# Loading an expert's first rows during the attention loop, and dropping the constant products before the experts

## The chip, the cores and the metric

The kernel runs on one core of a Trainium2 chip. A core has five engines with an instruction stream each: TensorE (PE in the profile, its weight loads PEld), VectorE (DVE), ScalarE (ACT), GpSimd (POOL) and SyncE (SP), which here only issues transfers. They share an on-chip memory (SBUF) and the matmul accumulators (PSUM), and meet at semaphores. 16 DMA engines move data to and from main memory. The metric is the device time of one execution in microseconds (us). The kernel before takes 883.68 us, the median of three runs (883.65 to 884.09).

## The reference

```python
scores = matmul(z, z.T) / S                  # per batch: 3072 x 64 times 64 x 3072
x = u * matmul(maximum(scores, 0)**2, v)     # 8 batches x 3072 rows x 256 columns

logits = x @ w_gate                          # 8 experts
e_i, gate_i = argmax(logits), softmax(logits)[argmax]
# rows in order: row i takes the next place of expert e_i while counts[e_i] < 768,
# rows that find their expert full give an output of zero
h = maximum(disp[e] @ w1[e], 0)              # 768 x 256 times 256 x 1024
y = h @ w2[e]                                # 768 x 1024 times 1024 x 256
out[i] = gate_i * y[e_i, place_i]            # for the rows that were kept
```

An expert takes 768 rows at most. Once all eight are full, every later row has an output of zero, and attention for it needn't be computed.

## The kernel before

The 24576 rows of x are computed in groups of 384 rows (GROUP, three tiles of 128), eight groups to a batch. Matmuls take fp32 numbers as pairs of fp16 numbers (high and low parts). The program has two parts.

**The attention loop.** Each engine runs the same loop over groups n (`attention_loop`, line 213). Group 0 is peeled off. In pass n, TensorE computes the attention of group n in 12 steps c (scores for three steps ahead at lines 612 and 613, weighted sums at 647 to 651), ScalarE and VectorE turn scores into weights (434, 438, 916, 922), and beside it the rows finished in the pass before are routed: VectorE splits them (1014), SP transposes them by DMA (`xT`, line 263, three transfers), TensorE takes the logits in step 3 (line 688, waiting for `loaded_xT`), VectorE finds each row's place (1050 to 1088) and GpSimd scatters the rows with their gate weight and row number into `disp` in main memory (line 352). VectorE also writes a flag into `ends`: zero once all experts are full. Every engine reads it (`load_end`, line 222), and the loop is left after step 5 of the pass that finds them full. With these inputs that is pass 18 of 64.

SP's pass, in its order: wait for the split rows, three `xT` transposes, load of `ubuf` (264), in each eighth pass the next batch's z and v (277, 282) and a wait for them, in passes 1 to 8 zeros over an eighth of the output (298, 3 MB each), in passes 3 and 5 the weights of experts 0 and 1 (252, 254), a wait for `ubuf`, `load_end`, and in the last pass a wait until all scatters have landed. All of SP's transfers go through one DMA queue (q1 in the profile).

**The experts.** `disp` holds 16 halves of 384 rows, two for each expert. After the loop SP loads the first four (`load_rows`, 313): 384 rows transposed into `xt[:, k]` (line 315), then their gate weights and row numbers into `tail` (317). `xt` and `tail` lie in `vS`, which attention reads until its end, so that SP waits for `pe_over` first. TensorE waits until all engines have left attention (`attention_over` is 3), then does `hidden` (763) and `output` (786 to 790) in turns: the first needs `loaded_x0`. ScalarE and VectorE split the hidden values, GpSimd scatters the results to `out`.

**Constant products.** `turn_over(times)` (line 616) multiplies an identity by ones into a spare part of PSUM, and nobody reads the result. There are 138 at the program's start, 44 after the last attention matmul (`close`) and 36 after the wait for the other engines.

Of the kernel before, what the change touches and what calls it, by code (L numbers as in the profile page):

```python
# [12 lines left out]
F32 = mybir.dt.float32  # L13
# [9 lines left out]
P = 128  # L23
# [20 lines left out]
def relu2_attention_moe(nc, u, v, z, w_gate, w1, w2, out, disp, capacity):  # L44
# [12 lines left out]
    with ExitStack() as ctx:  # L57
# [12 lines left out]
        vS = sb("vS", [P, 2 * CHUNK, 2 * D], F16)  # L70
        rawv = sb("rawv", [P, CHUNK, D], F32)
        rawz = sb("rawz", [P, S // 2], F32)
        zsq = sb("zsq", [P, S // 2], BF16)
        attn = sb("attn", [P, BUFS, 2, GROUP], F32)
        attn_hi = sb("attn_hi", [P, BUFS, 2, GROUP], F16)
# [43 lines left out]
        row = sb("row", [P, 1], F32)  # L119
        least = sb("least", [P, 1], F32)  # L120
        ends = sb("ends", [1, NG], I32)

        identf = sb("identf", [P, P], F32)
        identh = sb("identh", [P, P], F16)
        before = sb("before", [P, P], F16)
        ones = sb("ones", [P, P], F16)
# [16 lines left out]
        fac = sb("fac", [P, 4, TILES], F32)  # L143

        over_s = vS[:, :, :].rearrange("p c d -> p (c d)")
        xt = over_s[:, 0:4 * 2 * DC * GROUP].rearrange("p (b m n) -> p b m n", b=4, m=2 * DC)
        tail = over_s.bitcast(F32)[:, 4 * DC * GROUP:4 * DC * GROUP + 4 * TILES * 2].rearrange(
            "p (b t d) -> p b t d", b=4, t=TILES)
        blank = over_s.bitcast(F32)[:, BLANK_AT * D:BLANK_AT * D + FILL_ROWS * XW].rearrange("p (r d) -> p r d", r=FILL_ROWS)
# [28 lines left out]
        def y_part(t):  # L178
# [11 lines left out]
            wpart_ready wmax_ready wallmax_ready wscale_ready whi_ready wlo_ready w_step  # L190
            loaded_x0 loaded_x1 loaded_x2 loaded_x3 loaded_t0 loaded_t1 loaded_t2 loaded_t3
            h_ready hh_done hl_done y_summed y_ready y_scattered0 y_scattered1 y_scattered2
            y_scattered3 fac_ready h_first hh_first"""
        s = {n: sem(n) for n in names.split()}
        consts = s["consts"]

# [42 lines left out]
        @block.sync  # L239
        def _(sp):  # L240
            for h in range(2):
                sp.dma_start(rawz[:, h * SLICE * P:(h + 1) * SLICE * P], z[0, :, h * SLICE * P:(h + 1) * SLICE * P]
                             ).then_inc(s[f"loaded_z0{h}"], 16)
            for q, name in enumerate("abcde"):
                sp.dma_start(rawv[:, V0_PIECES[q]:V0_PIECES[q + 1], :], v[0, :, V0_PIECES[q]:V0_PIECES[q + 1], :]
                             ).then_inc(s["loaded_v0" + name], 16)
            sp.wait_ge(s["loaded_v0e"], 16)
            sp.dma_start(wg[:, :, :], w_gate).then_inc(s["loaded_wg"], 16)

            def load_expert(e, par):  # L250
                e = e & (E - 1)
                sp.dma_start(wraw1[par][:, :, :], w1[bass.ds(e, 1), :, :].rearrange("a (c p) f -> p (a c) f", p=P)
                             ).then_inc(s[f"loaded_w{par}"], 16)
                sp.dma_start(wraw2[:, par, :, :], w2[bass.ds(e, 1), :, :, :].rearrange("a p c d -> p (a c) d")
                             ).then_inc(s[f"loaded_w{par}"], 16)

            def body(n, end):
                g = n & 7
                if not isinstance(n, int):

                    for t in range(TILES):
                        wait_apart(sp, s["rows_lo"], n * TILES - TILES + 1 + t)
                        sp.dma_start_transpose(xT[:, t, :, :], halves[:, t, 0:2 * D]).then_inc(s["loaded_xT"], 16)
                sp.dma_start(ubuf[:, :, :], u[bass.ds(n & (NG - 1), 1), :, :, :].rearrange("a p t d -> p (a t) d")
                             ).then_inc(s["loaded_u"], 16)
                def load_batch():

                    nxt = ((n + 8) & 56) // 8
                    for key in ("khi_ready", "klo_ready"):  # L270
                        if isinstance(n, int):
                            sp.wait_ge(s[key], 8)
                        else:
                            wait_apart(sp, s[key], (n & 120) + 8)
                    if not isinstance(n, int):
                        wait_apart(sp, s["split_ready"], (n & 120) + 8)
                    sp.dma_start(rawz[:, :], z[bass.ds(nxt, 1), :, :].rearrange("a p n -> p (a n)")
                                 ).then_inc(s["loaded_zv"], 16)
                    for q in range(SLICES):
                        if isinstance(n, int):  # L280
                            sp.wait_ge(s["split_ready"], 2 * q + 2)
                        sp.dma_start(rawv[:, q * SLICE:(q + 1) * SLICE, :],
                                     v[bass.ds(nxt, 1), :, q * SLICE:(q + 1) * SLICE, :].rearrange("a p c d -> p (a c) d")
                                     ).then_inc(s["loaded_zv"], 16)
                    wait_apart(sp, s["loaded_zv"], (n & 120) * 10 + 80)
                if isinstance(n, int):
                    rows = E * capacity // P
                    dv = disp.rearrange("(p r) d -> p r d", p=P)
                    sp.wait_ge(s["blank_ready"], 1)
                    for q in range(rows // FILL_ROWS):  # L290
                        sp.dma_start(dv[:, q * FILL_ROWS:(q + 1) * FILL_ROWS, :], blank
                                     ).then_inc(s["disp_filled"], 16)
                only_if(sp, g == 0, load_batch)
                if not isinstance(n, int):
                    def zero_out():

                        rows = B * S // 8
                        sp.dma_start(out[bass.ds(((n - 1) & 7) * rows, rows), :].rearrange("(p r) d -> p r d", p=P),
                                     empty[:, 0:D].unsqueeze(1).to_broadcast([P, rows // P, D])
                                     ).then_inc(s["out_zeroed"], 16)  # L300
                    only_if(sp, n <= 8, zero_out)
                if not isinstance(n, int):
                    only_if(sp, n == 3, lambda: load_expert(0, 0))
                    only_if(sp, n == 5, lambda: load_expert(1, 1))
                wait_apart(sp, s["loaded_u"], n * 16 + 16)
                load_end(sp, n, end)
                if not isinstance(n, int):
                    only_if(sp, sp.snap(end) < 1, lambda: wait_apart(sp, s["scattered"], n * 48))
                    only_if(sp, n == NG, lambda: sp.wait_ge(s["scattered"], NG * 48))
            attention_loop(sp, body)  # L310
            sp.wait_ge(s["pe_over"], 1)

            def load_rows(at, k):

                sp.dma_start_transpose(xt[:, k, :, :], disp_halves[bass.ds(at, GROUP), 0:2 * D]
                                       ).then_inc(s[f"loaded_x{k}"], 16)
                sp.dma_start(tail[:, k, :, :], disp[bass.ds(at, GROUP), D:D + 2].rearrange("(t p) d -> p t d", p=P)
                             ).then_inc(s[f"loaded_t{k}"], 16)

            for k in range(4):  # L320
                load_rows(k * GROUP, k)
            with sp.Fori(0, E // 2 - 1) as i:
                for k in range(4):
                    j = i * 4 + k
                    if k % 2 == 0:

                        wait_apart(sp, s["wlo_ready"], (i * 2 + k // 2 + 1) * 4)
                        load_expert(i * 2 + k // 2 + 2, k // 2)

                    wait_apart(sp, s[f"y_scattered{k}"], i * 48 + 48)  # L330
                    load_rows((j + 4) * GROUP, k)
# [249 lines left out]
        def _(pe):  # L581
# [54 lines left out]
            def body(n, end, par):  # L636
# [76 lines left out]
                def close():  # L713

                    for t in range(TILES):
                        nc.tensor.matmul(o_part(t), attn_hi[:, END_AT % BUFS, 0, t * P:(t + 1) * P],
                                         vS[:, par * CHUNK + END_AT, 0:D], start=False, stop=True,
                                         skip_group_check=True)
                    turn_over(44)
                    for register in (stop0, stop1, stop):  # L720
                        pe.reg_mov(register, 0)
                both_parts(pe, n, end, part, close)
# [17 lines left out]
            pe.drain().then_inc(s["pe_over"], 1)  # L740
            pe.sem_inc(s["attention_over"], 1)
            pe.wait_ge(s["attention_over"], 3)
            turn_over(36)

            pe.sem_inc(s["y_summed"], TILES)

            def hidden(i, k, p):
# [12 lines left out]
                for fi in range(2):  # L760
                    f = 2 * p + fi
                    for at, (w, x, m) in enumerate(terms):
                        ins = nc.tensor.matmul(Sp[:, 2 * (p % 2) + fi, 0:GROUP], w[par][:, m, f * P:(f + 1) * P],  # L763
                                               xt[:, k, x + m, :], start=(at == 0), stop=(at == len(terms) - 1))
                    if isinstance(q, int) and q == 0 and fi == 0:
                        ins.then_inc(s["h_first"], 1)
                ins.then_inc(s["h_ready"], 1)
# [45 lines left out]
        def _(dve):  # L813
# [17 lines left out]
                    for r in range(0, P, 32):  # L831
                        dve.tensor_scalar(row[r:r + 32, :], quad[r:r + 32, 0:1], float(r), None, ALU.add)
            dve.tensor_scalar(identh[:, :], col, row[:, 0:1], None, ALU.is_equal)
            dve.tensor_scalar(identf[:, :], col, row[:, 0:1], None, ALU.is_equal)
            dve.tensor_scalar(before[:, :], col, row[:, 0:1], None, ALU.is_gt)
            for t in range(TILES):
                dve.tensor_scalar(xrow[:, t, D + 1:D + 2].bitcast(I32), row[:, 0:1], float(t * P - GROUP), None, ALU.add)
# [131 lines left out]
            def body(n, end):  # L969
# [21 lines left out]
                def part(start, stop):  # L991
                    for c in range(start, stop):
# [18 lines left out]
                        if not peeled and c == ROWS_LO_AT:  # L1011
                            for t in range(TILES):
# [2 lines left out]
                                                               scalar=rscale[:, t:t + 1], in1=halves[:, t, 0:D],  # L1015
                                                               op0=ALU.mult, op1=ALU.subtract)
                                ins.then_inc(s["rows_lo"], 1)
                        if peeled and c == GATE_AT[0]:
                            dve.wait_ge(s["loaded_wg"], 16)
                            dve.tensor_reduce(gmx[:, :], wg[:, :, :], AX.XY, ALU.max, apply_absolute_value=True  # L1020
# [240 lines left out]
RSCALE_AT = 0  # L1261
ROWS_HI_AT = 1
ROWS_LO_AT = 0
LOGITS_AT = (3, 2)
COUNTS_AT = (4, 1)
EXP_AT = 4
# [59 lines left out]
```

## Time and profile before

| what | value |
| --- | --- |
| median of three runs | 883.68 us |
| profiled execution, its time | 883.7 us |
| its span, first to last instruction | 881.9 us |
| TensorE busy | 863.2 us, 98% of the span |
| VectorE busy | 631.5 us, 72% |
| ScalarE busy | 573.5 us, 65% |
| attention loop ends (last weighted sum) | about 616 us |
| experts begin (first hidden matmul) | 624.8 us |

The 1.8 us between the profiled execution's time and its span lie outside the span. "Busy" of TensorE holds the constant products too. A share of busy time says little here: what counts is who is waited for at a place.

### The profile page before, as it was taken

Reading aid. Unit: us, or ns where it says so; the run is one execution under the profiler, and the core shown is the slowest. Engines: PE = TensorE matmul, PEld = TensorE weight load, DVE = VectorE, ACT = ScalarE, POOL = GpSimd, SP = SyncE. Lnnn points to the kernel's source line nnn. Section 1 sums busy time; section 2 is a strip of 40 time slices with the busy share of each in tenths; the row PEclk is TensorE's granted clock in tenths of the full one; section 3 lists DMA queues with packets and bytes.
Section 4 is the critical chain, followed back from the end, with each engine's and each line's share of the span. In section 5 each row is a group of like instructions: output and inputs, shape, how many; then the busy total and the mean of one; then the engine's idle time right before and its main releaser. Section 6 shows DMA issues by size and latency. Waiting matters only on the chain.

```text
span 881.9 us, 22816 instructions
## 1 busy us (share of the span) xinstructions
PE 863.2 (98%) x7373; PEld 689.7 (78%) x7374; DVE 631.5 (72%) x1346; ACT 573.5 (65%) x874; POOL 122.5 (14%) x121
## 2 busy tenths in 40 slices
PE   6999999999999999999999999999899999999997
PEld 5887887888888887888888888888577777777776
DVE  7976777888888888788788887777265665655531
ACT  6968786768768669787777876776154444434422
POOL 0001101101101110110110110110012112121212
PEclk9999999999999999999999999999999999999999
DMA  8833625635642750110121013311714235325100
GB/s 297 335 101 132 196 83 208 196 96 195 196 126 77 258 155 23 42 50 22 36 54 36 18 52 86 138 42 36 171 37 151 56 129 167 101 77 155 54 18 36
DMA packets 101014, 97.85 MB, mean 111 GB/s; under 512 B 63885, under 2 KB 88538, under 8 KB 99968
## 3 DMA queue, kind: packets, MB, share of 16 engines
q1 hardware_dynamic: 96096, 84.92, 31.4%
q0 software_dynamic: 4896, 12.64, 4.0%
q8 instruction: 13, 0.21, 0.1%
q14 instruction: 9, 0.07, 0.0%
HBM read 40.03 MB, written 44.93 MB: 96 GB/s over the span
## 4 chain that ended last, share of the span: by engine, by line
PE 91%; DVE 3%; issue 3%; ACT 1%; DMA 1%; POOL 0%; ACTq 0%; DVEq 0%; POOLq 0%; SPq 0%
PE O L647 15%; PE O L651 15%; PE O L649 15%; PE Sc L763 14%; PE Sc L612 8%; PE Sc L613 8%; PE O L786 3%; PE O L788 3%; PE O L790 3%; PE M L788 2%; PE M L786 2%; PE M L790 2%; PE M L688 1%; DVE attn_hi L916 0%; ACT Sc L434 0%
## 5 line engine op out<-in xcount | busy, mean ns | idle before, releaser
L647 PE MATMUL O<-vS,attn_hi 128*128 128x256 f16 x1332 | 363.0, 273 | 1.8 <-DVE vS L905 1.6
L651 PE MATMUL O<-vS,attn_lo 128*128 128x256 f16 x1332 | 363.1, 273 | 0.0
L649 PE MATMUL O<-vS,attn_hi 128*128 128x256 f16 x1332 | 363.0, 273 | 0.0
L434 ACT ACTIVATE Sc<-Sc 128x768 f32<-128x768 f32 x224 | 177.9, 794 | 93.1 <-PE Sc L613 72.0
L922 DVE TENSOR_TENSOR attn_lo<-attn,attn_hi 128x768 f16<-128x768 f32 x224 | 214.7, 958 | 7.7
L438 ACT ACTIVATE attn<-Sc 128x768 f32<-128x768 f32 x224 | 181.6, 811 | 7.1
L647 PEld LDWEIGHTS O<-vS,attn_hi 128*128 128x128 f16 x1332 | 130.3, 98 | 29.1 <-issue 1.8
L649 PEld LDWEIGHTS O<-vS,attn_hi 128*128 128x128 f16 x1332 | 130.3, 98 | 26.5
L612 PE MATMUL Sc<-zP 128*128 (+1 forms) x450 | 146.5, 326 | 3.4 <-issue 2.1
L916 DVE CAST attn_hi<-attn 128x768 f16<-128x768 f32 x224 | 125.0, 558 | 32.5 <-ACT attn L438 28.3
L613 PE MATMUL Sc<-zQ,zP 128*128 (+1 forms) x450 | 146.4, 326 | 0.0
L651 PEld LDWEIGHTS O<-vS,attn_lo 128*128 128x128 f16 x1332 | 130.3, 98 | 15.2
L1216 DVE SCALAR_TENSOR_TENSOR rawv<-Sc,rawv 128x768 f16<-128x768 f32 x63 | 60.2, 956 | 114.1 <-ACT rawv L543 72.0
L352 POOL DMA_INDIRECT disp<-xrow,slot x54 | 69.4, 1285 | 475.9 <-DVE slot L1087 442.2
L543 ACT ACTIVATE rawv<-Sc 128x768 f16<-128x768 f32 x63 | 51.0, 810 | 101.1 <-PE Sc L763 98.4
L763 PE MATMUL Sc<-vS,w1h 128*128 128x384 f16 x512 | 105.4, 329 | 2.3 <-DMA vS<-disp 2.3
L763 PEld LDWEIGHTS Sc<-vS,w1h 128*128 128x128 f16 x512 | 50.4, 99 | 31.2 <-DMA vS<-disp 2.5
L786 PE MATMUL O<-w2s,rawv 128*128 128x256 f16 x256 | 69.8, 273 | 0.0
L790 PE MATMUL O<-w2s,rawv 128*128 128x256 f16 x256 | 69.8, 273 | 0.0
L788 PE MATMUL O<-w2s,rawv 128*128 128x256 f16 x256 | 69.8, 273 | 0.0
L387 POOL DMA_INDIRECT out<-attn,vS x48 | 46.9, 977 | 123.1 <-ACT attn L555 109.3
L612 PEld LDWEIGHTS Sc<-zP 128*128 128x128 f16 (+1 forms) x450 | 43.9, 98 | 24.0 <-issue 6.0
(151 smaller groups left out, 890.4 us busy)
## 6 DMA issues: line engine op xcount, KB each, us to landing
out<-empty SPq DMA_DIRECT2D x8, 3072.0 KB, 12.0
wraw<-in_moe_w SPq DMA_DIRECT2D x16, 1024.0 KB
rawv<-in_v SPq DMA_DIRECT2D x14, 768.0 KB, 7.5
ubuf<-in_u SPq DMA_DIRECT2D x19, 384.0 KB, 3.1
disp<-vS SPq DMA_DIRECT2D x8, 774.0 KB, 9.2
rawz<-in_z SPq DMA_DIRECT2D x3, 768.0 KB
xT<-xrow SPq DMA_TRANSPOSE x54, 2.4
disp<-xrow,slot POOLq DMA_INDIRECT x54
```

The costliest lines, as they stand in the source:

```text
L434: act.activation(pair, pair, ACT.Relu).then_inc(s["relu_done"], 1)
L438: act.activation(attn[:, c % BUFS, :, :], Sp[:, 2 * (c % 2):2 * (c % 2) + 2, 0:GROUP], ACT.Square, scale=ROOT_C).then_inc(s["square_done"], 1)
L612: nc.tensor.matmul(to, keys, zP[:, bass.ds(qb, GROUP)], start=True, stop=False)
L613: ins = nc.tensor.matmul(to, keys, zQ[:, bass.ds(qb, GROUP)], start=False, stop=True)
L647: nc.tensor.matmul(o_part(t), hi, v[:, 0:D], start=c == 0 and j == 0 and t % 2 == 0, stop=False, skip_group_check=True)
L649: nc.tensor.matmul(o_part(t), hi, v[:, D:2 * D], start=False, stop=False, skip_group_check=True)
L651: ins = nc.tensor.matmul(o_part(t), lo, v[:, 0:D], start=False, stop=c == PAIRS - 1 and j == 1, skip_group_check=True)
L763: ins = nc.tensor.matmul(Sp[:, 2 * (p % 2) + fi, 0:GROUP], w[par][:, m, f * P:(f + 1) * P], xt[:, k, x + m, :], start=(at == 0), stop=(at ...
L786: nc.tensor.matmul(y_part(t), hi, w2s[:, par, f, 0:D], start=f == 0, stop=False, skip_group_check=True)
L788: nc.tensor.matmul(y_part(t), hi, w2s[:, par, f, D:2 * D], start=False, stop=False, skip_group_check=True)
L916: dve.tensor_copy(attn_hi[:, b, :, :].rearrange("p j n -> p (j n)"), attn[:, b, :, :].rearrange("p j n -> p (j n)")).then_inc(s["hi_done"], 1)
L922: dve.tensor_tensor(attn_lo[:, b, :, :], attn[:, b, :, :], attn_hi[:, b, :, :], ALU.subtract).then_inc(s["lo_done"], 1)
```

## The change

A buffer `x0` of its own takes the rows of expert 0's first half. SP loads it in every pass from 1 on, at the end of the pass's transfers, and waits for the load. Ahead of the load it waits until as many scatters have landed as the register `due` says. VectorE writes that number in step 1 of each pass: 48 for each earlier pass (a pass scatters three tiles, 16 counts each), and 48 more if expert 0 still had under 384 rows when this pass began. The last pass's load is the one that is used. After the loop SP only raises `loaded_x0`, and then loads tail 0 and the rows and tails of halves 1 to 3 as before. The wait for the last scatters stands behind the loop. The 44 and 36 constant products are gone (the 138 at the start stay), and so is `identf`, a second identity that no instruction reads.

```diff
+        x0 = sb("x0", [P, 2 * DC, GROUP], F16)
...
-        identf = sb("identf", [P, P], F32)
...
-        xt = over_s[:, 0:4 * 2 * DC * GROUP].rearrange("p (b m n) -> p b m n", b=4, m=2 * DC)
+        xt = [x0[:, :, :]] + [over_s[:, b * 2 * DC * GROUP:(b + 1) * 2 * DC * GROUP].rearrange("p (m n) -> p m n", m=2 * DC)
+                              for b in range(1, 4)]
...
                 wait_apart(sp, s["loaded_u"], n * 16 + 16)
+                if not isinstance(n, int):
+
+                    wait_apart(sp, s["due_ready"], n * 2)
+                    sp.reg_load(due, dues[0:1, bass.ds((n - 1) & (NG - 1), 1)])
+                    wait_apart(sp, s["scattered"], sp.snap(due))
+                    sp.reg_mov(due, n * 48)
+                    sp.dma_start_transpose(x0[:, :, :], disp_halves[0:GROUP, 0:2 * D]).then_inc(s["loaded_early"], 16)
+                    wait_apart(sp, s["loaded_early"], n * 16)
                 load_end(sp, n, end)
-                if not isinstance(n, int):
-                    only_if(sp, sp.snap(end) < 1, lambda: wait_apart(sp, s["scattered"], n * 48))
-                    only_if(sp, n == NG, lambda: sp.wait_ge(s["scattered"], NG * 48))
...
             attention_loop(sp, body)
+            sp.sem_inc(s["loaded_x0"], 16)
+            wait_apart(sp, s["scattered"], sp.snap(due))
             sp.wait_ge(s["pe_over"], 1)
...
-            for k in range(4):
+            load_tail(0, 0)
+            for k in range(1, 4):
                 load_rows(k * GROUP, k)
...
-                    turn_over(44)
...
-            turn_over(36)
-
             pe.sem_inc(s["y_summed"], TILES)
...
-            dve.tensor_scalar(identf[:, :], col, row[:, 0:1], None, ALU.is_equal)
...
+                        if not peeled and c == DUE_AT:
+
+                            dve.tensor_scalar(lacking[:, :], base[0:1, 0, 0:1], float(GROUP), 48.0, ALU.is_lt, ALU.mult
+                                              ).then_inc(s["due_ready"], 1)
+                            dve.wait_ge(s["due_ready"], n * 2 - 1)
+                            dve.scalar_tensor_tensor(out=dues[0:1, bass.ds((n - 1) & (NG - 1), 1)],
+                                                     in0=xrow[0:1, 0, D + 1:D + 2].bitcast(I32), scalar=48.0 / GROUP,
+                                                     in1=lacking[:, :], op0=ALU.mult, op1=ALU.add
+                                                     ).then_inc(s["due_ready"], 1)
...
+DUE_AT = 1
```

SP's stream from the wait for `ubuf` to the first load behind the loop, before (ISA and the ALU rows are waits and register work, `ends` is the flag):

```order
L201 ISA
L227 REGISTER_ALU x2
L227 ISA
L227 TENSOR_LOAD ends
L210 COMPARE_AND_BRANCH
L201 REGISTER_ALU
L210 UNCONDITIONAL_BRANCH
L210 COMPARE_AND_BRANCH
L210 UNCONDITIONAL_BRANCH
L219 REGISTER_ALU
L219 COMPARE_AND_BRANCH
L315 DMA_TRANSPOSE vS<-disp 128x4x384
```

The same stretch after (the lines of the changed kernel are numbered otherwise, and `x` is `x0`):

```order
L204 ISA
L204 REGISTER_ALU
L312 REGISTER_ALU x2
L312 ISA
L312 TENSOR_LOAD dues
L314 ISA
L315 DMA_TRANSPOSE x<-disp 128x4x384
L230 REGISTER_ALU
L230 TENSOR_LOAD ends
L222 REGISTER_ALU
L222 COMPARE_AND_BRANCH
L327 DMA vS<-disp 128x3x2
```

The row load now stands inside the loop, ahead of the flag's read, and is run in every pass; the first transfer behind the loop is tail 0.

TensorE's stream from the closing attention matmuls to the first hidden ones, before:

```order
L716 MATMUL O<-vS,attn_hi 128x256 x3
L619 MATMUL O<-ones,identh 128x128 x44
L235 UNCONDITIONAL_BRANCH
L737 REGISTER_ALU
L737 COMPARE_AND_BRANCH
L736 UNCONDITIONAL_BRANCH
L739 ISA
L727 COMPARE_AND_BRANCH
L619 MATMUL O<-ones,identh 128x128 x36
L763 MATMUL Sc<-vS,w1h 128x384 x4
L763 MATMUL Sc<-vS,w1l 128x384 x2
```

And after:

```order
L733 MATMUL O<-vS,attn_hi 128x256 x3
L238 UNCONDITIONAL_BRANCH
L753 REGISTER_ALU
L753 COMPARE_AND_BRANCH
L752 UNCONDITIONAL_BRANCH
L755 ISA
L743 COMPARE_AND_BRANCH
L777 MATMUL Sc<-x,w1h 128x384 x4
L777 MATMUL Sc<-x,w1l 128x384 x2
```

Between the last attention matmul and the first hidden one there are now only branches and waits.

## Rows read from the trace of the kernel before

**Rows 1.** The chain that ended last, end of attention: start, us, what.

```profile
618.61 2.10 DMA disp<-xrow,slot
...
621.15 3.59 DMA vS<-disp
...
624.78 7.63 PE Sc L763 x36
634.38 1.95 PE Sc L763 x12
```

**Rows 2.** Timeline of PE: start, us, instruction, idle before and its releaser.

```profile
616.04 0.49 PE L716 MATMUL O<-vS,attn_hi 128*128 128x256 f16 x3
616.37 2.62 PE L619 MATMUL O<-ones,identh 128*128 128x128 f16 x44
620.27 2.18 PE L619 MATMUL O<-ones,identh 128*128 128x128 f16 x36 [1.29 <-PEq L741]
624.78 1.46 PE L763 MATMUL Sc<-vS,w1h 128*128 128x384 f16 x4 [2.33 <-DMA vS<-disp]
```

**Rows 3.** Windows: us, busy PE to POOL, granted clock, DMA share, GB/s.

```profile
622.50:624.50 2.00, 0.00 (x0) 0.00 (x0) 0.00 (x0) 0.00 (x0) 0.00 (x0) 1.00 1.01 198
616.00:620.00 4.00, 2.98 (x49) 2.76 (x47) 1.42 (x2) 0.00 (x0) 2.97 (x3) 1.00 0.05 16
625.00:628.00 3.00, 3.00 (x11) 1.40 (x10) 0.41 (x1) 0.49 (x1) 0.00 (x0) 0.50 1.13 164
```

**Rows 4.** Lines on the sequencers, pass 18: min, median, max ns, first start.

```profile
L740 PEldq DRAIN  x1: 1107/1107/1107, 619.0 to 619.0; - x1
L1205 DVEq DRAIN  x1: 66/66/66, 617.4 to 617.4; - x1
L227 SPq TENSOR_LOAD <-ends x1: 280/280/280, 614.5 to 614.5; - x1
```

**Rows 5.** Timeline of SP: last pass, and first load behind the loop.

```profile
608.88 0.36 SPq L264 DMA_DIRECT2D ubuf<-in_u  x1
621.15 1.48 SPq L315 DMA_TRANSPOSE vS<-disp  x1
```

**Rows 6.** The page's DMA issues; at the end median us to landing.

```profile
ubuf<-in_u SPq DMA_DIRECT2D x19, 384.0 KB, 3.1
xT<-xrow SPq DMA_TRANSPOSE x54, 2.4
vS<-disp SPq DMA_TRANSPOSE x16, 3.7
```

**Rows 7.** Timeline of SP, passes 4, 8 and 9.

```profile
155.34 3.98 SPq L263 DMA_TRANSPOSE xT<-xrow  x3
...
305.39 0.64 SPq L298 DMA_DIRECT2D out<-empty  x1
316.80 3.97 SPq L263 DMA_TRANSPOSE xT<-xrow  x3
```

**Rows 8.** Windows of passes 3, 8 and 16; the DMA share is last but one.

```profile
137.00:138.00 1.00, 1.00 (x8) 0.61 (x7) 0.96 (x3) 0.00 (x0) 0.26 (x1) 1.00 0.99 267
315.00:316.00 1.00, 1.00 (x11) 0.90 (x10) 0.96 (x2) 1.00 (x4) 0.00 (x0) 1.00 0.78 252
561.00:573.00 12.00, 12.00 (x105) 10.00 (x103) 7.45 (x16) 9.39 (x18) 0.00 (x0) 1.00 0.00 0
```

**Rows 9.** Line 298 in pass 8: us from issue to landing.

```profile
DMA to landing us min/median/max: 12.2/12.2/12.2
```

**Rows 10.** Timeline of PE: the logits of pass 9.

```profile
322.19 0.45 PE L688 MATMUL M<-wgs,xT 128*128 128x16 f16 x12
```

**Rows 11.** Who waited for line 688: us, times, whole program.

```profile
DVE logit L1050: 18.7, 18
```

**Rows 12.** Timeline of DVE: the flag's write in pass 18.

```profile
614.01 0.14 DVE L1083 TENSOR_SCALAR ends<-least 1x1 f32 x1 [0.23 <-DVE posf L1081]
```

**Rows 13.** The chain at the program's start.

```profile
4.01 0.20 DVE identf L834
```

More of the change, by code:

```diff
@@ L121, in relu2_attention_moe @@
         ends = sb("ends", [1, NG], I32)
-        identf = sb("identf", [P, P], F32)
+        dues = sb("dues", [1, NG], I32)
+        lacking = sb("lacking", [1, 1], F32)
         identh = sb("identh", [P, P], F16)
@@ L192, in relu2_attention_moe @@
             h_ready hh_done hl_done y_summed y_ready y_scattered0 y_scattered1 y_scattered2
-            y_scattered3 fac_ready h_first hh_first"""
+            y_scattered3 fac_ready h_first hh_first due_ready loaded_early"""
         s = {n: sem(n) for n in names.split()}
@@ L305, in body, with load_tail, load_rows @@
                 wait_apart(sp, s["loaded_u"], n * 16 + 16)
+                if not isinstance(n, int):
[5 more added lines that the diff above has]
+                    wait_apart(sp, s["loaded_early"], n * 16)
                 load_end(sp, n, end)
-                if not isinstance(n, int):
-                    only_if(sp, sp.snap(end) < 1, lambda: wait_apart(sp, s["scattered"], n * 48))
-                    only_if(sp, n == NG, lambda: sp.wait_ge(s["scattered"], NG * 48))
+            due = sp.alloc_register("due_SP")
+            sp.reg_mov(due, 48)
             attention_loop(sp, body)
+            sp.sem_inc(s["loaded_x0"], 16)
+            wait_apart(sp, s["scattered"], sp.snap(due))
             sp.wait_ge(s["pe_over"], 1)
-            def load_rows(at, k):
-                sp.dma_start_transpose(xt[:, k, :, :], disp_halves[bass.ds(at, GROUP), 0:2 * D]
-                                       ).then_inc(s[f"loaded_x{k}"], 16)
+            def load_tail(at, k):
                 sp.dma_start(tail[:, k, :, :], disp[bass.ds(at, GROUP), D:D + 2].rearrange("(t p) d -> p t d", p=P)
                              ).then_inc(s[f"loaded_t{k}"], 16)
-            for k in range(4):
+            def load_rows(at, k):
+                sp.dma_start_transpose(xt[k], disp_halves[bass.ds(at, GROUP), 0:2 * D]
+                                       ).then_inc(s[f"loaded_x{k}"], 16)
+                load_tail(at, k)
+            load_tail(0, 0)
+            for k in range(1, 4):
                 load_rows(k * GROUP, k)
@@ L763, in hidden @@
                         ins = nc.tensor.matmul(Sp[:, 2 * (p % 2) + fi, 0:GROUP], w[par][:, m, f * P:(f + 1) * P],
-                                               xt[:, k, x + m, :], start=(at == 0), stop=(at == len(terms) - 1))
+                                               xt[k][:, x + m, :], start=(at == 0), stop=(at == len(terms) - 1))
                     if isinstance(q, int) and q == 0 and fi == 0:
```

## The prediction

> **What bounds the kernel now.** I read the page first: TensorE is busy for 98% of the span and the chain of waits is nearly all TensorE, so only its rate, its clock and its few gaps can pay. In the chain in order of time the one long stretch without TensorE lies between attention and the experts: the last scatter lands at 620.7 (618.61 and 2.10), the first rows are then loaded in 3.6 us, and the first hidden matmuls follow at 624.78 [rows 1]. The timeline of TensorE shows what it did meanwhile. Its last useful matmuls start at 616.04; up to 622.45 it works on constant products with a gap of 1.29 us, then it idles for 2.33 us on the load [rows 2]. So the end of attention isn't late for the load: the load waits for scatters, and 8.2 us of the span (616.58 to 624.78) hold nothing useful. The windows give the clock: granted 1.00 through 624.5, and 0.50 at 625 to 628 [rows 3], the lower level (1.2 GHz), after the 2.33 us idle.
>
> **The change part by part.**
>
> *Experts start earlier.* x0 is in place before the loop is left, and no scatter stands ahead of it. TensorE's first hidden matmul then waits for the last of three things. Its own exit: before, the last product ended at 618.98, the drain took 1.11 us from 619.0 [rows 4] and the next matmul started 1.29 us after the last one [rows 2]. The same behind the closing attention matmuls, which end near 616.58 (three at 0.11 apart from 616.04, the last with its 0.27): 617.87. VectorE's exit: its drain ends at 617.5 [rows 4], 0.4 us earlier. ScalarE left before both. SP's: `ubuf` issued at 608.88 lands 3.2 us later, at 612.1 [rows 5, 6]; register work and a read like that of `ends` (0.28 [rows 4]), some 0.7 us together, put the x0 load at 612.85; it lands 3.6 to 3.7 us later [rows 1, 6], 616.5; the read of `ends` and the loop's branches take another 0.8, so `loaded_x0` is raised at 617.3. That is 0.55 us ahead of TensorE. I take 617.87: 6.91 us gained. Bounds: no drain cost behind a short queue would give VectorE's 617.55 (7.2 gained); a load that takes 4.8 us instead of 3.6, as one of the four did in traffic behind the loop, gives 618.5 (6.3). What is late next: tail 0 and rows 1 leave SP at 621 as before, since the wait for scatters stays ahead of them. Rows 1 land by 626.5, and TensorE wants them after four hidden and two output blocks, 4 x 1.95 + 2 x 1.97 = 11.7 us after its start, at 629.6. VectorE's first row factors wait for tail 1 (near 626.7) with the next low part queued behind them; TensorE needs that part at 629.8 and it takes 1 us. Both are covered, with 2 to 3 us to spare.
>
 I take the whole 1.7 as gained; the other end is 0.
>
> *Constant products.* Their 2.62 and 2.18 us leave TensorE's stream. They were hidden behind the wait for the load, so they pay nothing beyond the terms above, where their absence already stands. What they might have guarded is the clock, priced as a rival.
>
> *The load in every pass.* It adds to SP a wait for `due`, a register read, a wait for scatters and a transfer of 393 KB whose landing is awaited. Queued behind it on SP are the next pass's `xT` transposes, and TensorE stands still in step 3 if these are late. In most passes there is room: in pass 18 SP was idle from 609 on, and in pass 16 the batch's load is over by 561 with SP idle till the next transposes at 572.85 (the DMA engines show 0.00 in between [rows 8]); zeros and weights of pass 3 keep the engines full to 145, the load would end near 148, and the next transposes go at 155.34 [rows 7]. In pass 8 there is no room. SP first waits for the batch, issues 3 MB of zeros at 305.39 and only then comes to x0, while the next transposes started at 316.80 [rows 7]. The zeros' traffic ends near 315.8 (share 0.78 in that microsecond [rows 8]) and they land at 317.6 [rows 9]. x0 stands behind them in one queue. In pass 3 the weights behind the zeros started with no gap (share 0.99 as the zeros run out [rows 8]), so I let x0 start at 315.8, not at 317.6. Alone, its traffic lasts 1.9 us (622.5 to 624.4, share 1.01 [rows 3]) and it lands 0.35 later: 318.05. With 0.95 for the read of `ends` and the branches, the transposes start at 319.0, 2.2 us late; three at 1.26 apart put the third at 321.6 and its landing, 2.4 later [rows 6], at 324.0. TensorE came to the logits at 322.15 [rows 10]. It idles 1.9 us, and nothing makes that up: VectorE's routing waits for those logits, and the scores that ScalarE wants next are queued behind them on TensorE. Bounds: 0 if x0 shares the engines with the zeros instead of queueing; 5.0 if it starts only at the zeros' landing (317.6 + 3.6 = 321.2, transposes at 322.15, the third lands at 327.15). An idle of 5 us would also cost 1.7 of clock, so 6.7.
>
> The page "DMA: Bandwidth & Descriptors" of the Trainium skill speaks to this in "Two DMAs through the same engine are not ordered": within a queue of a DMA engine transfers start in order but are pipelined, so the later one needn't wait for the earlier one's writes. By that rule the 0 and the 5.0 are both wrong and the 1.9 stands; pass 3's windows agree, and for a transpose behind zeros no row here shows it. The same page ("Latency and other measured facts") gives a transposing DMA 261 GB/s; for 393 KB an estimate from it is 1.5 us where this trace shows 1.9, and the stall would be 1.5 instead of 1.9, the sum 0.4 lower.
>
> *VectorE's two writes a pass.* The nearest row is the flag's write, 0.14 with 0.23 idle before it for its address [rows 12]: 0.14 + 0.23 + 0.14, about 0.5 us a pass, in step 1. VectorE then idles for the logits in step 3 anyway, 18.7 us in 18 passes, 1.04 each [rows 11], at least 0.8 where I looked. So 0 on the path. If that cover were gone it is 18 x 0.5 = 9 us; from below nothing is gained.
>
> *`identf`.* It stands for 0.20 us on the chain at the start [rows 13], which goes on through VectorE: 0.2 gained.
>
> **The sum,** made on the profiled execution (883.7 us, of which 1.8 lie outside the span; the median of the runs is 883.68, the same): 883.7 - 0.2 - 6.9 - 1.7 + 1.9 = **876.8 us**.
>
> **The rivals.**
>
> *A, the forecast:* 876.8, own range 875.6 to 878.2 from the start's bounds and half a microsecond on the stall. Chance 0.50.
>
> *B, no stall in pass 9* (x0 gets through beside the zeros, or SP's late transposes are made up): 883.7 - 0.2 - 6.9 - 1.7 = 874.9. For it: the engines do serve two queues at once. Against it: x0 and the zeros are in the same queue. 0.20.
>
> *C, the long stall* (x0 starts at the zeros' landing, and the clock falls in the gap): up to 874.9 + 6.7 = 881.6. For it: writes land 1.8 us after their traffic ends; against it: pass 3. 0.12.
>
> *D, the experts still begin at the low clock,* since 80 products that kept TensorE busy are gone: 876.8 + 1.7 = 878.5. For it: nothing but the gap's length speaks for the clock, and 1.29 and 2.33 are the only two seen. 0.12.
>
> *E, slower:* VectorE's writes are on the path, in step 1 of all 18 passes, because TensorE's next weighted sum waits for the low parts queued behind them: 876.8 + 9 = 885.8. It decides once VectorE's wait for the logits is under 0.5 us on average; it is 1.04 now. 0.04.
>
> *F, the change doesn't do what it says:* another wait, SP's or VectorE's, holds the first hidden matmul at 624.8. Then only the stall and `identf` are left: 883.7 + 1.9 - 0.2 = 885.4 if the clock falls again, 883.7 if it doesn't. Against it: both waits are over by 617.6 in the rows. 0.02.
>
> **How the numbers follow.** The likeliest is A, 876.8. The range 874.6 to 880.2 holds A, B and D and the milder half of C. About 0.2% (1.8 us) is what a measurement of this kernel can tell from no change. A to D are all faster by more than that (C at its worst by 2.1): 0.94, and I give 0.93 to leave some for a still longer stall; 0.02 for the same, from F and C's edge; 0.05 for slower, from E and the rest of F.
>
> **What would show it.** In the profile after, the first hidden matmul should start about 1.3 us behind the last attention matmul, with the granted clock at 1.00 there, and the last scatter should land while it runs. The experts' part should then be as long as before less 1.7 us. Pass 9 should show TensorE idle for about 2 us ahead of the logits, released by a transpose, with SP's three transposes some 2 us later after the loop's start than now; passes 2 to 8 and 10 to 18 should show none. VectorE's wait for logits should shrink by about 0.5 us a pass, and nothing else move. The prediction is wrong if another pass has such a gap, if the hidden matmuls run at 0.50 at the experts' start, or if TensorE waits for low parts in steps 2 to 4.

## The result, and the profile after

| | median | runs |
| --- | --- | --- |
| before | 883.66 us | 881.99 to 884.09, 4 runs |
| changed | 875.96 us | 875.40 to 877.52, 4 runs |
| predicted | 876.8 us | 874.6 to 880.2 |

The ratio is 0.9919 (95% interval 0.9901 to 0.9937): the medians differ by 7.7 us, and the interval gives 5.6 to 8.7. Both kernels have two levels of time within these ranges, which go with TensorE's clock and are told below.

The profiled execution of the changed kernel is its slowest run, 877.5 us with a span of 875.7. The chain of waits at the end of attention (start, us, what), against [rows 1]:

```profile
618.35 0.56 DVE attn_hi L929
619.05 0.30 DVEq L230
...
620.25 6.01 PE Sc L777 x36
...
628.22 1.95 PE Sc L777 x12
```

Neither a scatter nor a load is in it any more, and 36 hidden matmuls take 6.01 us instead of 7.63. TensorE's timeline, against [rows 2]:

```profile
618.57 0.49 PE L733 MATMUL O<-vS,attn_hi 128*128 128x256 f16 x3
620.25 0.81 PE L777 MATMUL Sc<-x,w1h 128*128 128x384 f16 x4 [1.18 <-DVEq L1227]
```

From the last closing attention matmuls to the first hidden one it is 1.68 us start to start, where it was 8.74. The windows (stretch, us, busy by engine, granted clock, DMA share, GB/s) answer to [rows 3] with the clock at 1.00; the first scatter of the last pass was issued at 617.8 and the last at 621.05, so the last one lands while the hidden matmuls run:

```profile
620.00:625.00 5.00, 4.75 (x30) 2.91 (x31) 1.11 (x2) 1.64 (x3) 1.72 (x2) 1.00 0.08 11
625.00:628.00 3.00, 3.00 (x26) 2.36 (x25) 1.09 (x2) 0.96 (x2) 0.00 (x0) 1.00 1.10 173
```

The sequencers in the last pass, against [rows 4]:

```profile
L757 PEldq EVENT_SEMAPHORE  x1: 51/51/51, 619.2 to 619.2; - x1
L222 SPq COMPARE_BRANCH  x1: 45/45/45, 619.6 to 619.6; - x1
L1227 DVEq DRAIN  x1: 66/66/66, 619.9 to 619.9; - x1
```

TensorE had left the loop at 619.2, SP at 619.65, and VectorE was last at 619.95. And SP's timeline where pass 8 meets pass 9, and in pass 18, against [rows 5, 7]:

```profile
304.33 0.62 SPq L301 DMA_DIRECT2D out<-empty  x1
307.11 7.03 SPq L315 DMA_TRANSPOSE x<-disp  x1
318.29 3.89 SPq L266 DMA_TRANSPOSE xT<-xrow  x3
...
611.37 0.37 SPq L267 DMA_DIRECT2D ubuf<-in_u  x1
615.49 1.48 SPq L315 DMA_TRANSPOSE x<-disp  x1
```

In pass 8 the early load's issue alone takes 7.03 us behind the zeros, elsewhere 1.3 to 1.5. Passes 1 to 7 have the same 3 MB of zeros, but there the load is issued 12.9 to 17.6 us behind them, and the zeros land 11.3 to 12.3 us from their issue. In pass 2, for instance, `due` was read at 96.8, the last scatter was issued at 103.0 and the load went at 107.35: with expert 0's first half not yet full, the load waits for the scatters of its own pass. In pass 8 the batch delays zeros and load, the scatters have landed by then, and the load goes 2.8 us behind the zeros. The transposes of pass 9 start at 318.29; those of passes 2 to 8 had all started earlier than before (283.32 against 284.17 for pass 8). TensorE's timeline and the windows show what follows, against [rows 8, 10]:

```profile
323.57 0.47 PE L705 MATMUL M<-wgs,xT 128*128 128x16 f16 x12 [2.37 <-DMA xT<-xrow]
```

```profile
315.00:316.00 1.00, 1.00 (x11) 0.85 (x10) 1.00 (x4) 0.97 (x3) 0.00 (x0) 1.00 1.23 278
316.00:317.00 1.00, 1.00 (x10) 0.75 (x9) 0.97 (x3) 1.00 (x2) 0.00 (x0) 1.00 0.60 132
317.00:318.00 1.00, 1.00 (x12) 0.90 (x10) 0.84 (x2) 0.97 (x2) 0.00 (x0) 1.00 0.00 0
322.00:323.00 1.00, 0.00 (x0) 0.00 (x0) 0.00 (x0) 0.00 (x0) 0.00 (x0) 1.00 0.64 131
324.00:327.00 3.00, 3.00 (x16) 1.86 (x13) 1.80 (x11) 1.83 (x3) 0.00 (x0) 0.54 0.26 102
```

TensorE idles 2.37 us for the transposes of pass 9, and in this run the clock falls to 0.50 as the gap ends (0.66 granted in 323 to 324), for 3.4 us.

The account of the two profiled executions, by the start of SP's transposes in each pass (the lists begin 56.98 before and 56.52 after):

| stretch | before to after |
| --- | --- |
| up to pass 1 | -0.46 |
| passes 1 to 8 | -0.39 (284.17 and 283.32 at its end) |
| pass 8 to 10, gap and clock | +3.52 (349.30 and 351.97) |
| passes 10 to 18 | -0.14 (604.69 and 607.22) |
| pass 18 to the first hidden matmul | -7.06 (20.09 and 13.03) |
| first 36 hidden matmuls | -1.62 (7.63 and 6.01) |
| sum, of 6.18 in the span | -6.15 |

### The profile page after: what moved, and what is told of

The parts are those of the page before. It is cut to its first block, busy times and chain, and to the rows that moved or that the text cites. A ratio compares the mean times of both kernels' runs of the same rounds, so it can differ in the third digit from the quotient of the medians.

```text
span 875.7 us, 22817 instructions
## 1 busy us (share of the span) xinstructions
PE 858.0 (98%) x7293; PEld 684.7 (78%) x7294; DVE 635.4 (73%) x1381; ACT 573.9 (66%) x874; POOL 123.4 (14%) x121
## 4 chain that ended last, share of the span: by engine, by line
PE 89%; DMA 3%; issue 2%; DVE 2%; SPq 1%; ACT 1%; ACTq 0%; POOL 0%; DVEq 0%; POOLq 0%
PE O L664 15%; PE O L668 15%; PE O L666 15%; PE Sc L777 14%; PE Sc L629 8%; PE Sc L630 7%; PE O L800 3%; PE O L804 3%; PE O L802 3%; PE M L804 2%; PE M L802 2%; PE M L800 2%; DMA rawv<-in_v 1%; DMA x<-disp 1%; SPq L266 1%
## 5 line engine op out<-in xcount | busy, mean ns | idle before, releaser
L777 PE MATMUL Sc<-vS,w1h 128*128 128x384 f16 x384 | 78.1, 326 | 0.0
L630 PEld LDWEIGHTS Sc<-zQ,zP 128*128 128x128 f16 (+1 forms) x450 | 44.0, 98 | 17.1 <-issue 0.2
```

The source lines that it names most:

```text
L630: ins = nc.tensor.matmul(to, keys, zQ[:, bass.ds(qb, GROUP)], start=False, stop=True)
```

## The experiments

**Is it the early load of pass 8 that makes pass 9 late, and do the other loads cost anything?** The load is left out in passes 1 to 8:

```diff
-                    wait_apart(sp, s["due_ready"], n * 2)
...
-                    wait_apart(sp, s["loaded_early"], n * 16)
+                    with sp.If(n > 8):
+                        load_early()          # the same steps
+                    with sp.Else():
+                        sp.sem_inc(s["loaded_early"], 16)
```

> The changed kernel with the early load left out in passes 1 to 8 (the semaphore is raised instead). Theory Q (in pass 8 the load queues behind 3 MB of zeros, which makes the next pass's transposes late; the loads of the other passes cost nothing): TensorE has no gap before the logits of pass 9, the clock stays at 1.00 there, and the time is 2.4 us (the gap) below the best runs of the changed kernel, near 873.3 us, and as much as 3.5 us below the profiled one. Rival R1 (each early load costs a little, through the DMA engines that it shares): more than that is gained, as 8 of 18 loads are gone. Rival R2 (the gap comes from pass 8's batch load or from VectorE, not from the early load): the gap stays and the time is that of the changed kernel, 876.0.

Measured: 873.97 us (873.91 to 874.04, 4 runs), ratio 0.9896 (0.9881 to 0.9911). SP's timeline, and the window around pass 9's logits:

```profile
304.18 0.62 SPq L301 DMA_DIRECT2D out<-empty  x1
315.51 3.98 SPq L266 DMA_TRANSPOSE xT<-xrow  x3
```

```profile
310.00:325.00 15.00, 14.97 (x140) 12.03 (x139) 13.40 (x44) 10.47 (x21) 0.00 (x0) 1.00 0.55 157
```

The transposes go at 315.51 instead of 318.29, TensorE has no gap and the clock stays. It takes 2.0 us off the changed kernel's median, and with the gap its spread: four runs within 0.13 us. R2 is out. The expected 873.3 was too low by 0.7. Part of it is lost again at the experts' start, 13.42 us behind pass 18's transposes here against 13.03 in the changed kernel.

**Do the zeros in the queue matter, or the batch ahead of them?** A first attempt moved the zeros of passes 1 to 8 to passes 2 to 9, which leaves those of pass 8 where they are:

```diff
-                    only_if(sp, n <= 8, zero_out)
+                    only_if(sp, n > 1, lambda: only_if(sp, n <= 9, zero_out))
```

> The changed kernel with all 18 early loads, but the eight zero transfers issued in passes 2 to 9 instead of 1 to 8. Pass 9's early load then queues behind zeros too, but no batch is loaded in that pass, so there is time. Wait: pass 8 still has its zeros, behind the batch, so this moves only which pass is last; theory Q says that the gap ahead of pass 9's logits stays at 2.4 us, that pass 10 has none, and that the time is that of the changed kernel (876.0, 0.5 either way). A rival in which the first pass matters (the zeros of pass 1 against the fill of the buffer) would show a different start: under 0.5 us.

Measured: 877.15 us (875.77 to 878.28, 5 runs). The gap stayed, 2.26 us in the profiled run, and pass 10 has none. The median missed the expected 876.0 within 0.5; in four of the five runs the mean clock was 0.998 or less. The transposes from pass 2 on also start 0.7 us earlier (88.48 against 89.18), more than the 0.5 allowed, so that the zeros of pass 1 cost something there. On the question asked the run tells little, since pass 8 kept both its batch and its zeros. The second moves only those of pass 8:

```diff
-                    only_if(sp, n <= 8, zero_out)
+                    only_if(sp, n <= 7, zero_out)
+                    only_if(sp, n == 9, lambda: zero_out(7))     # the same eighth of the output
```

> The changed kernel with all 18 early loads, and the zeros of pass 8 issued in pass 9 instead (zeros in passes 1 to 7 and 9). Theory Q (the queue behind the zeros): no gap ahead of the logits of pass 9 or 10, clock 1.00 there, time that of the kernel that loads from pass 9 on, 874.0 within 0.3. Rival R1 (each early load costs a little): 874.0 plus a visible amount for the 8 loads of passes 1 to 8. Rival R3 (it is the batch load ahead of it, not the zeros, that makes pass 8 late): the gap of 2.4 us stays, 876 or more.

Measured: 874.21 us (874.14 to 874.37, 4 runs), 0.9886 (0.9871 to 0.9901). SP's timeline in passes 8 to 10:

```profile
305.12 1.47 SPq L317 DMA_TRANSPOSE x<-disp  x1
315.52 3.89 SPq L266 DMA_TRANSPOSE xT<-xrow  x3
...
320.68 0.61 SPq L302 DMA_DIRECT2D out<-empty  x1
324.31 7.08 SPq L317 DMA_TRANSPOSE x<-disp  x1
348.54 2.58 SPq L266 DMA_TRANSPOSE xT<-xrow  x2
```

With all 18 loads and the same batch load the gap is gone. The load behind zeros now takes 7.08 us to issue in pass 9, where nothing waits for it. So the queue behind the zeros is the cause, shown from both sides. The loads of passes 1 to 7 cost nothing: pass 8's transposes start at 283.22 here and at 283.19 without these loads. The 0.2 us between the medians (874.21 against 873.97, on two chips) lies elsewhere: pass 9, which now has the zeros, takes 0.6 us longer here (348.54 against 347.92 at the start of pass 10's transposes).

**The spread of the changed kernel,** run again unchanged.

> The changed kernel unchanged, to see how its time spreads over runs on one chip. Theory: in runs whose mean granted clock is 1.000 or 0.999 the gap ahead of pass 9's logits leaves the clock alone and the time is 875.4 to 876.0; in runs at 0.998 or less the clock falls after the gap and the time is 1.5 us more. Rival: the spread comes from elsewhere and doesn't go with the clock.

Measured: 876.89 us (875.48 to 877.78, 5 runs). With the clock at 0.999: 875.48 and 875.96; at 0.998 or 0.997: 876.89, 877.52 and 877.78. The two levels are there as expected, with 0.9 to 2.3 us between them where 1.5 was expected. In the profiled run of these (875.96) TensorE idles the same 2.37 us before pass 9's logits, and the granted clock is 1.00 in 323 to 327. Its pass 10 starts 67.26 us behind pass 8 (350.41 and 283.15), where it was 65.13 before and 68.65 in the run whose clock fell: the gap costs 2.13 us by itself and the clock 1.39 more. The kernel before has two levels too: of 43 runs beside these experiments, 20 with the clock at 0.999 or 1.000 have a median of 882.4, 21 at 0.997 or 0.998 one of 884.1, and two at 0.996 took 886.4 and 886.8. In its profiled run (0.997) the fall is at the experts' start, behind the wait for the load; no run of the upper clock was profiled, so that for those it is inferred that the clock stayed there. Compared level with level, the change is worth 6.5 us (882.4 to 875.9) and 6.6 us (884.1 to 877.5). The 7.7 between the first medians holds about 1 us of chance, since by their times three of the first four runs of the kernel before were on its slower level, and three of the four of the changed kernel on its faster one.

**The constant products.** Back in the changed kernel, 44 behind the closing matmuls and 36 behind the wait:

```diff
+                    turn_over(44)
...
             pe.wait_ge(s["attention_over"], 3)
+            turn_over(36)
```

> The changed kernel with the 44 and 36 constant products back in their places. If what the change gains at the end of attention is held only by TensorE's own stream, the products cost their length: 2.6 us for the 44 (they run past VectorE's exit by 1.7) and 2.2 us for the 36, so the experts start 3.9 to 4.8 us later than in the changed kernel and the time is about 880.3. The clock at the experts' start is 1.00 either way. Rival: they guard the clock there, and without them some runs lose 1.7 us; then the difference is 1.7 us smaller in such runs.

Measured: 884.17 us (881.63 to 885.34, 11 runs), 1.0009 (0.9999 to 1.0019), and TensorE's timeline:

```profile
620.04 2.62 PE L636 MATMUL O<-ones,identh 128*128 128x128 f16 x44
623.80 2.18 PE L636 MATMUL O<-ones,identh 128*128 128x128 f16 x36 [1.14 <-PEq L758]
```

From pass 18's transposes to the end of the span it is 273.0 us, against 268.5 in the changed kernel: 4.5 us for the products, within the expected 3.9 to 4.8. The time came out higher than expected. The gap of pass 9 is 3.2 us in its trace rather than 2.4, and ten of eleven runs have the clock at 0.998 or less; the one at 1.000 took 881.63. The longer gap follows the zeros of pass 8, which took 12.3 us to land instead of 11.3, with 8.24 us for the early load's issue behind them; why they took longer stays open. And the kernel before with the products taken out, the two `turn_over` lines alone:

> The kernel before without its 44 and 36 constant products, nothing else changed. The load of the first rows still sets the experts' start, so theory says the start stays at 624.8 and the time at 883.7, give or take the clock: TensorE now idles 8.2 us there instead of 2.3, the clock is at 0.50 when it starts, and the loss is between 0.8 and 1.7 us as before. Rival (the products themselves cost time): 2 to 5 us less.

Measured: 884.30 us (883.59 to 884.94, 11 runs), 1.0011 (1.0000 to 1.0021). TensorE's timeline and windows:

```profile
624.68 1.46 PE L761 MATMUL Sc<-vS,w1h 128*128 128x384 f16 x4 [8.29 <-DMA vS<-disp]
```

```profile
616.00:624.00 8.00, 0.39 (x4) 0.10 (x1) 1.28 (x2) 0.00 (x0) 2.84 (x3) 0.82 0.26 58
625.00:630.00 5.00, 5.00 (x23) 2.62 (x22) 1.12 (x2) 0.98 (x2) 0.00 (x0) 0.70 1.12 165
```

The start stays at 624.7, and now the mean clock is 0.994 to 0.996 in every run; in the profiled one it falls already within the wait. So ahead of a long wait the products are free and keep the clock up in about half the runs; behind an early load they cost their length.

**Is it the rule of when to load, or only its place in the loop?** In the kernel that loads from pass 9 on, the load of a pass always waits for that pass's own scatters:

```diff
-                        wait_apart(sp, s["scattered"], sp.snap(due))
                         sp.reg_mov(due, n * 48)
+                        wait_apart(sp, s["scattered"], sp.snap(due))
```

> The kernel that loads from pass 9 on, but the early load of a pass always waits for that pass's own scatters too (the number that VectorE writes is read and not used). It takes away only that the load may go ahead once expert 0's half is full. Theory: the last scatter lands at 619.15 in that kernel's trace, the load 3.7 us later and SP's reading and branches 0.8 after that, so the experts start at 623.8 instead of 616.6, and after 8 us of idling at the low clock (1.7 lost): 874.0 + 7.2 + 1.7 = 882.9. Rival (the gain came from the load's place in the loop or the missing products, not from its being ahead of the scatters): 874 to 876.

Measured: 883.21 us (882.90 to 883.90, 10 runs), 1.0004 (0.9994 to 1.0013). SP's and TensorE's timelines:

```profile
619.15 1.46 SPq L316 DMA_TRANSPOSE x<-disp  x1
```

```profile
623.81 1.46 PE L782 MATMUL Sc<-x,w1h 128*128 128x384 f16 x4 [8.81 <-SPq L326]
```

The experts start 20.66 us behind pass 18's transposes, where it was 20.09 before and 13.42 with the early rule. So all of the gain at the experts' start is in going ahead of the last scatters. In all ten runs the mean clock is 0.994 or 0.995, and what the other parts of the change gained goes into that.

**VectorE's two writes a pass,** taken out of the kernel that loads from pass 9 on:

> The kernel that loads from pass 9 on, without VectorE's two writes in each pass; SP waits for the scatters of all earlier passes instead, which with these inputs is what the written number comes to from pass 9 on. Theory: VectorE idles for the logits in every pass, so its two writes are free and the time is 874.0 within 0.3. Rival E (they are on the path, 0.4 us in 18 passes): 7 us less, near 867.

Measured: 874.63 us (874.53 to 874.86, 4 runs). E is out: without the writes nothing is gained. The time also missed the expected 874.0 within 0.3, on the other side. The kernel that loads from pass 9 on, which differs in the writes and SP's use of them alone, took 873.97 and 873.76 (on other chips), so 0.7 to 0.9 us is lost without the writes. The traces agree: pass 18's transposes start at 604.11 here and at 603.22 and 603.06 there, and nearly all of it has built up by pass 10 (348.74 against 347.92 and 347.83).

**`identf`** built again in the kernel that loads from pass 9 on, and that kernel itself beside it:

> The kernel that loads from pass 9 on, with VectorE's second identity built again at the start. Theory: it stands on the chain there for 0.20 us, so 874.2 and the first transposes of pass 1 go 0.2 us later. Rival (its removal also closed the gap of 0.49 us that the chain showed after 11.13 before and 0.25 us now, so 0.46 was gained by pass 1): 874.4.

> The kernel that loads from pass 9 on, unchanged, on the same chip as the two kernels beside it: 874.0 within 0.2 in every run, with the clock at 1.000 or 0.999 throughout, whatever the kernel before does between its two levels (882.2 to 882.9 with the clock at 0.999, 883.7 to 884.4 at 0.998 or less).

Measured: 874.19 us (873.89 to 874.42, 4 runs) and 873.76 us (873.44 to 874.60, 4 runs). SP's first transposes, with `identf` and without:

```profile
56.98 1.28 SPq L267 DMA_TRANSPOSE xT<-xrow  x1
```

```profile
56.54 1.45 SPq L266 DMA_TRANSPOSE xT<-xrow  x1
```

The rival was right: 0.44, not 0.20. The chain with `identf` has the gap of 0.49 us at 11.13 again, where the changed kernel's has 0.25 at 10.93. Of the repeated kernel's four runs one (873.95) lay within the 0.2 expected: 873.44 and 873.58 were below, and 874.60, at a clock of 1.000, above. What made that run slower is open. The clock was at 0.999 or 1.000 in all four, as expected.

**Who sets the experts' start now?** In the kernel that loads from pass 9 on, TensorE waits for ScalarE alone, and SP issues the load ahead of its wait for `ubuf`:

```diff
             act.drain().then_inc(s["attention_over"], 1)
+            act.sem_inc(s["act_over"], 1)
...
-            pe.wait_ge(s["attention_over"], 3)
+            pe.wait_ge(s["act_over"], 1)
...
-                wait_apart(sp, s["loaded_u"], n * 16 + 16)      # now behind the early load
```

> The kernel that loads from pass 9 on, with two waits loosened at the end of attention: TensorE starts the experts when ScalarE has left attention instead of waiting for VectorE too, and SP issues the early load ahead of its wait for ubuf, 2 us earlier. In the changed kernel's trace VectorE's drain at 619.9 released TensorE, whose own drain was over at 619.2, and SP raised its semaphore at 619.7. Theory V (VectorE's exit sets the start): the experts start 0.7 to 0.9 us earlier, 873.2. Rival P (TensorE's own drain and branches set it, as the prediction had it, 1.29 us behind the last matmul): 874.0, unchanged.

Measured: 872.92 us (872.84 to 873.08, 4 runs), 0.9871 (0.9856 to 0.9887), the fastest version here. TensorE's timeline and its drain:

```profile
614.49 0.49 PE L741 MATMUL O<-vS,attn_hi 128*128 128x256 f16 x3
615.56 0.81 PE L785 MATMUL Sc<-x,w1h 128*128 128x384 f16 x4 [0.57 <-issue]
```

```profile
L764 PEldq DRAIN  x1: 108/108/108, 614.9 to 614.9; - x1
```

P is out: TensorE's own exit takes 0.57 us of idling, and its drain 0.11 where it was 1.11 before [rows 4]. It is 0.93 in the changed kernel with the products back and 0.01 in the kernel before without them, so the products make the difference.

V is only half shown, since two waits were loosened at once. In the profile of the changed kernel and of its repeat VectorE was the last, as V has it. In three others SP was: with the zeros in passes 2 to 9, with `identf`, and in the repeat of the very kernel that this experiment starts from, where SP raised `loaded_x0` at 616.2, VectorE's drain ended at 615.8 and TensorE started at 616.28. In these five traces the two lie 0.5 us apart at most, so that loosening one wait alone should gain no more than that; it wasn't run. Together they gave 0.8 to 1.0 us (872.92 against 873.76 and 873.97).

## Why the prediction was right, step by step

*Experts start earlier, 6.9 us.* 7.06 in the traces. Its mechanism is shown (waiting for the own scatters gives these 7 us back). But the reason given for the start was wrong: the prediction let TensorE's own drain and branches set it, 1.29 us behind the last matmul, as [rows 2] had it. That drain of 1.11 us belonged to the stream with 44 products; without them it is 0.10, and VectorE's exit came last. That the number held is luck: TensorE's exit was put too late and VectorE's too early, for from the end of its drain to the first hidden matmul another 0.29 us passed, and the two forecasts lay 0.3 us apart. SP was to be 0.55 us ahead of TensorE; it was 0.5 behind it, and only 0.3 ahead of VectorE. From the landing of `ubuf`, 3.1 us from its issue, to the early load it took 1.0 us, not 0.7.

*The clock, 1.7 us.* 1.62 in the traces, and 1.00 at the experts' start in both profiles. It is right for that pair of executions only. About half the runs of before don't show the loss, and there it isn't gained; that the sum starts from 883.7, a run with the low clock, was luck too. D didn't occur in any run of the kernels without a gap in pass 9 (24 runs, all at 0.999 or 1.000).

*The load in pass 8, 1.9 us lost.* 2.37 of idling for the predicted reason, in the predicted pass and in no other. The transposes went at 318.29; forecast were 319.0, less the 0.85 gained by then, 318.15. The landing of the third came some 0.4 later than reckoned. The share is 1.23 in 315 to 316 as the zeros run out, with no pause, and the traffic ends at 316.6. The zeros landed at 315.6 (11.3 us from their issue), and a load of 1.9 us of traffic that starts there would end at 317.5 at the earliest. By this the rule of the Trainium skill's page "DMA: Bandwidth & Descriptors" ("Two DMAs through the same engine are not ordered"), that transfers of one queue start in order but are pipelined, agrees with the trace. The rate for a transposing DMA on the same page of the Trainium skill ("Latency and other measured facts") would have made the stall shorter, and it was longer. What the forecast left out in its likeliest case, and had only in C, is the clock behind this gap: by the mean clock it fell in one of the four first runs and in three of the five of the repeat. Its own cost is 1.4 us (3.52 less the 2.13 of the run whose clock stayed).

*VectorE's writes, 0.* VectorE's wait for the logits fell from 18.7 to 12.3 us:

```profile
DVE logit L1072: 12.3, 18
```

The two writes take 0.13 and 0.15 us with 0.22 of waiting between them, 0.5 a pass as reckoned. The wait shrank by 0.36 a pass, less than the 0.5 forecast, and nothing was lost by them; by the experiment without them they go with a gain of 0.7 to 0.9 us.

*`identf`, 0.2.* 0.44: a start 0.2 us earlier also halved a wait further down the chain.

*Not forecast:* 0.39 us gained in passes 1 to 8 and 0.14 later. The kernel without VectorE's writes doesn't show this gain (its transposes of pass 8 go at 283.79), the ten traces of kernels that have them do (283.08 to 283.57, but for the kernel with zeros from pass 2 on, 282.46). How the writes would do that isn't shown.

*The sum.* With the terms as measured and the clock kept, as in A, it is 883.7 - 0.46 - 0.39 - 0.14 - 7.06 - 1.62 + 2.13 = 876.2, and the profiled run of the repeat, whose clock stayed, took 875.96. So the forecast's 876.8 is close because its terms are close; `identf` (0.3) and the unforeseen 0.5 us in passes 1 to 18 make most of the rest. It forecast one level; the changed kernel has two, 875.9 and 877.5, and its median lies on the first or the second by chance (875.96 in the first four runs, 876.89 in the repeat).

Of the rivals, C's clock happened with A's gap in some runs; B, E and F are out by the traces and experiments above.

## What to carry to other kernels

A load that waits for the last of many small writes can go ahead of them when its own part is known to be complete; count what it needs, and check what else is waited for at that place: here TensorE, SP and VectorE left attention within 0.8 us, so a further gain there needs all three. A transfer whose landing is awaited has to be looked at in every pass of the loop, not in the typical one: in one queue it costs nothing seventeen times, and makes a gap of 2.4 us the one time that it is issued right behind 3 MB. Filler work that keeps the clock up was worth its place here only ahead of a wait longer than itself. And where a kernel has two levels of time, compare level with level: a median of four runs can lie on either.

## What the runs showed of the hardware that was not expected

A drain of TensorE took 1.11 and 0.93 us behind the 44 constant products and 0.01 to 0.13 us in the kernels without them, so its length in a trace belongs to what stands ahead of it, not to the instruction.

A single DMA issue on SP took 7.0 to 8.2 us right behind a transfer of 3 MB, and 1.3 to 1.5 us alone: SP was held at the issue, before any wait. That the queue was full is the likely reason, but no row shows it.

The clock fell behind a gap of 2.4 us in one profiled run and not in another of the same kernel; where it fell behind gaps of 2.3 to 3.2 us, it was at 0.50 for 3.4 us (three traces). By the mean clock, none of the 24 runs without a gap over 1.6 us had a fall, and all 21 with one of 8 us had.
